# An early tile for expert 0 in a fused attention, mixture-of-experts and Fourier-mixing kernel

## What is computed

```
B, S, D, E, F = 2, 768, 512, 8, 1024         # batches, tokens, width, experts, hidden width
x = attention(q, k, v)                       # 8 heads of 64; first 8 keys and a window of 96
logits = x @ w_gate;  keep = sigmoid(x @ w_local) >= 0.5
for each batch b, for each token s in order:
    e = argmax(logits[b, s]) if s == 0 or not keep[b, s] else the expert of token s - 1
    y[b, s] = softmax(logits[b, s])[e] * (relu(x[b, s] @ w1[e]) @ w2[e])
u = y + real(fft(fft(y, over tokens), over width))
out = u + relu(normalised(u) @ w_ch1) @ w_ch2          # w_ch1: 512 x 2048
```

## Time and profile before

| what | value |
|---|---|
| median of 3 runs | 678.57 us (677.31 to 679.86) |
| the profiled execution's own time | 677.65 us |
| its span | 675.8 us |
| PE busy | 649.7 us (96%) |
| DVE, ACT, POOL busy | 317.0, 207.5, 213.7 us |
| HBM over the span | 122 GB/s |

### The profile page before, as it was taken

One profiled execution on the slowest core, in us unless ns is written; L12 is line 12 of the kernel. 1 busy time (PEld: TensorE's weight loads), 2 busy tenths in 40 slices (PEclk: granted clock), 3 DMA queues, 4 the chain that ended last, 5 costly groups with the idle time before them and its releaser, 6 DMA issues.

```text
span 675.8 us, 10507 instructions
## 1 busy us (share of the span) xinstructions
PE 649.7 (96%) x3372; PEld 530.2 (78%) x3373; DVE 317.0 (47%) x828; ACT 207.5 (31%) x410; POOL 213.7 (32%) x120
## 2 busy tenths in 40 slices
PE   8999999769999999999998989999999999999997
PEld 7777878658888888888875668888888888888886
DVE  4999787574635446345347845441221111311112
ACT  3666544303332432433204752132211122111110
POOL 0000001235778777999515646270000000000000
PEclk9999999879999999999999989999999999999999
DMA  8664347226657556678255033210010000100001
GB/s 300 245 223 165 130 132 283 81 114 236 212 166 270 191 188 243 219 243 272 64 182 163 17 125 124 94 32 0 1 62 1 1 0 1 63 0 1 0 1 62
DMA packets 35409, 82.91 MB, mean 123 GB/s; under 512 B 3362, under 2 KB 7714, under 8 KB 35364
## 3 DMA queue, kind: packets, MB, share of 16 engines
q1 hardware_dynamic: 17952, 40.46, 16.8%
q10 hardware_dynamic: 15492, 35.56, 15.9%
q0 software_dynamic: 1920, 6.29, 2.8%
HBM read 67.35 MB, written 14.94 MB: 122 GB/s over the span
## 4 chain that ended last, share of the span: by engine, by line
PE 85%; DVE 9%; issue 2%; DMA 2%; ACT 1%; POOL 0%; DVEq 0%; ACTq 0%; POOLq 0%; SPq 0%
PE psum L597 22%; PE psum L599 22%; PE psum L598 22%; PE psum L1888 5%; PE psum L1860 3%; PE psum L1871 2%; PE psum L2036 2%; PE psum L1798 2%; PE psum L1996 1%; DVE prob L1407 1%; DMA bounds_i<-in_n_local 1%; PE psum L1792 1%; DVE prob_t L1421 1%; PE psum L2117 1%; DMA u<-y_sorted,result_rows 1%
## 5 line engine op out<-in xcount | busy, mean ns | idle before, releaser
L722 POOL TENSOR_TENSOR w<-raw,w 128x1024 fp32r<-128x1024 f32 x56 | 132.5, 2398 | 40.0 <-ACT w L820 39.8
L1752 DVE SCALAR_TENSOR_TENSOR act_t<-psum,act_t 128x512 fp32r<-128x512 f32 x48 | 33.2, 691 | 191.6 <-ACT act_t L1102 191.6
L820 ACT ACTIVATE w<-raw 128x1024 fp32r<-128x1024 f32 x64 | 67.3, 1058 | 123.9 <-PE psum L599 55.7
L1102 ACT ACTIVATE act_t<-psum 128x512 fp32r<-128x512 f32 x48 | 28.7, 598 | 217.8 <-PE psum L599 217.8
L597 PE MATMUL psum<-un_t,wc 128*128 128x512 f32 x192 | 75.5, 393 | 1.4 <-DVE un_t L1676 1.4
L597 PE MATMUL psum<-wc,act_t 128*128 128x512 f32 x192 | 75.6, 394 | 0.0
L599 PE MATMUL psum<-un_t,wc 128*128 128x512 f32 x192 | 75.4, 393 | 0.0
L598 PE MATMUL psum<-un_t,wc 128*128 128x512 f32 x192 | 75.2, 392 | 0.0
L599 PE MATMUL psum<-wc,act_t 128*128 128x512 f32 x192 | 74.8, 390 | 0.0
L598 PE MATMUL psum<-wc,act_t 128*128 128x512 f32 x192 | 74.8, 389 | 0.0
L874 ACT ACTIVATE prob<-prob,top 128x256 f32<-128x256 f32 (+1 forms) x96 | 46.2, 482 | 48.1 <-DVE top L1407 47.7
(11 more groups left out here) (273 smaller groups left out, 1109.9 us busy)
## 6 DMA issues: line engine op xcount, KB each, us to landing
raw<-in_moe_w ACTq DMA_DIRECT2D x60, 512.0 KB, 4.3
k_win<-in_k SPq DMA_DIRECT2D x8, 768.0 KB, 5.6
raw<-in_moe_w_ch SPq DMA_DIRECT2D x12, 512.0 KB, 3.3
v_win<-in_v SPq DMA_DIRECT2D x8, 704.0 KB, 4.2
xs<-x_sorted SPq DMA_DIRECT2D x17, 256.0 KB, 4.6
y_sorted<-ys SPq DMA_DIRECT2D x16, 256.0 KB, 3.4
q_t<-in_q SPq DMA_DIRECT2D x8, 384.0 KB, 3.5
out<-u SPq DMA_DIRECT2D x12, 256.0 KB, 2.0
```

The source lines that it names most:

```text
L722: nc.gpsimd.tensor_tensor(w[:, slot, 1, m, at_:at_ + PIECE], raw[:, n % RING, :], w[:, slot, 0, m, at_:at_ + PIECE].bitcast(f32), ALU.subt ...
L820: nc.scalar.activation(w[:, slot, 0, m, at_:at_ + PIECE], raw[:, n % RING, :], ACT.Copy).then_inc(high_done, 1)
L1102: nc.scalar.activation(act_t[n % 2][:, 0, :], bank(act_bank(n)), ACT.Relu).then_inc(act_high, 1)
L1752: nc.vector.scalar_tensor_tensor(act_t[n % 2][:, 1, :], bank(act_bank(n)), 0.0, act_t[n % 2][:, 0, :].bitcast(f32), ALU.max, ALU.subtract) ...
```

## The change

The first 128 tokens of batch 0 for expert 0 (or all of them, if there are fewer) become tile 0. They have 128 rows of their own at the head of x_sorted, cleared at the program's start. The areas of the experts begin 128 rows later, and expert 0's area holds only what is beyond the first 128 of batch 0, and batch 1's tokens. There may be two more tiles than before (SLOTS). SP loads tile 0 as soon as batch 0's six scatters have landed (first_scattered), without the row numbers of control.

PE turns tile 0 ahead of the last two gate sums of batch 1. Its up products are put between the five routing steps of batch 1: 9 before turn_flags, 3 before ends_to_row, 3 before carry_to_column, 9 behind rank_tokens. Then come its 8 transposes and 18 of the 24 down products, 6 filler calls, the wait for the control words and 6 more. The other 6 down products stand behind the turning of tile 1. The fillers and waits that stood there before are gone, and the two register loads are behind first_up(1, 1). ACT writes the high parts and rectifies the hidden tile (first_tile_high, first_tile_hidden). DVE writes the low parts: first_tile_low ahead of the logits of batch 1, first_tile_rest inside control behind base_row, and first_tile_result copies the result after x_tile(1, 1). DVE has four more small operations in place(0), of which two are before the slots, and one in place_results. The three last gate sums have another bank, and the buffers xs, xs_t and hid0 have other places. The diff, cut to its core (the helpers turn_tile, up, first_up and tile_step of PE are moved up unchanged, but for second_product, which is taken out of tile_step):

```diff
-SLOTS = NT + E
+SLOTS = NT + E + 2
...
+    first_row = AREA * np.arange(E) + 2 * P
     row = np.concatenate([
         np.tile(slope, B),
         E - np.arange(E),
-        AREA * np.arange(E) + P,
+        np.where(np.arange(E) > 0, first_row, P),
+        first_row,
...
+    hid = [None, rc("hid1", [P, F])]
+
+    assert route_start <= rc.next and rc.next + 12288 <= rg.next
+    x2_at = rc.next
     xs = [rc(f"xs{n}", [P, DM]) for n in range(2)]
     xs_t = [rc(f"xs_t{n}", [P, 2, NC, P], f32r) for n in range(2)]
-    hid = [rc(f"hid{n}", [P, F]) for n in range(2)]
+    hid[0] = rc("hid0", [P, F])
...
-        BANK_LAST = bank(0)[:, 0:ST * (E + 1)]
+        BANK_LAST = bank(7)[:, 2 * P:2 * P + ST * (E + 1)]
...
+
+            sp.wait_ge(zeros_ready, 1)
+            sp.dma_start(x_sorted[0:P, :], zeros[:, :]).then_inc(first_tile_cleared, 16)
...
-            sp.wait_ge(zeros_ready, 1)
...
-            sp.wait_ge(rows_ready, 1)
...
-            first_rows = [row_of(j) for j in range(2)]
...
-            sp.wait_ge(scattered, 16 * NT)
-            for par in range(2):
-                load_tile(first_rows[par], par)
+            sp.wait_ge(first_scattered, 16 * ST)
+            sp.dma_start(xs[0][:, :], x_sorted[0:P, :]).then_inc(xs_loaded[0], 16)
+            sp.wait_ge(rows_ready, 1)
+            first_rows = [row_of(j) for j in range(1, 3)]
+            sp.wait_ge(scattered, 16 * ST)
+            load_tile(first_rows[0], 1)
             sp.wait_ge(xs_turned, 1)
-            load_tile(row_of(2), 0)
+            load_tile(first_rows[1], 0)
...
+            pool.wait_ge(first_tile_cleared, 16)
...
-                                        x_att[:, t, :], None).then_inc(scattered, 16)
+                                        x_att[:, t, :], None).then_inc(first_scattered if t < ST else scattered, 16)
...
+            def first_tile_high():
+                act.wait_ge(xs_turned, 1)
+                nc.scalar.activation(xs_t[0][:, 0, :, :].rearrange("p c n -> p (c n)"), bank(4), ACT.Copy
+                                     ).then_inc(xs_t_high, 1)
+
+            def first_tile_hidden():
+                for part in range(2):
+                    act.wait_ge(hid_sum, part + 3)
+                    nc.scalar.activation(hid[0][:, part * 512:(part + 1) * 512], bank(part), ACT.Relu
+                                         ).then_inc(hid_ready, 1)
+                act.wait_ge(hid_turned, 1)
+                for z in range(2):
+                    nc.scalar.activation(hid_t[:, 0, 4 * z:4 * z + 4, :].rearrange("p c n -> p (c n)"), bank(2 + z),
+                                         ACT.Copy).then_inc(hid_t_high, 1)
...
+                first_tile_high()
...
             gate_exponentials(1)
+            first_tile_hidden()
...
-            for n in range(2):
-                act.wait_ge(xs_loaded[n], 16)
+            act.wait_ge(xs_loaded[1], 16)
+            act.wait_ge(xs_loaded[0], 32)
...
+                if b == 0:
+                    link(nc.vector.tensor_scalar(in_first_tile[:, :], slot_f[:, these], 2.0 * P, float(P), ALU.is_lt,
+                                                 ALU.mult))
+                    link(nc.vector.tensor_tensor(slot_f[:, these], slot_f[:, these], in_first_tile[:, :],
+                                                 ALU.subtract))
                 nc.vector.tensor_copy(slots[:, these], slot_f[:, these]).then_inc(slots_ready, 1)
                 if b == 0:
                     link(nc.vector.tensor_tensor(area[:, :], row["area"], upto[0][:, :, ST - 1], ALU.add))
+                    link(nc.vector.tensor_tensor(area[:, :], area[:, :], row["first_row"], ALU.max))
+                    link(nc.vector.tensor_tensor(sorted_first[:, :], area[:, :], row["first_row"], ALU.subtract))
                 else:
-                    link(nc.vector.tensor_tensor(count[:, :], upto[0][:, :, ST - 1], upto[1][:, :, ST - 1], ALU.add))
+                    link(nc.vector.tensor_tensor(count[:, :], sorted_first[:, :], upto[1][:, :, ST - 1], ALU.add))
...
+                    rows = by_token[:, 0, b * ST:(b + 1) * ST]
+                    link(nc.vector.tensor_reduce(rows, cand[:, :, :], AX.X, ALU.add))
+                    if b == 0:
+                        link(nc.vector.scalar_tensor_tensor(rows, in_first_tile[:, :], 0.0, rows, ALU.is_equal,
+                                                            ALU.mult))
...
+            def first_tile_low():
+                dve.wait_ge(xs_t_high, 1)
+                flat_ = [xs_t[0][:, x, :, :].rearrange("p c n -> p (c n)") for x in (0, 1)]
+                nc.vector.tensor_tensor(flat_[1], bank(4), flat_[0].bitcast(f32), ALU.subtract
+                                        ).then_inc(xs_t_ready, 1)
+
+            def first_tile_rest():
+                for z in range(2):
+                    hi, lo = (hid_t[:, x, 4 * z:4 * z + 4, :].rearrange("p c n -> p (c n)") for x in (0, 1))
+                    dve.wait_ge(hid_t_high, z + 1)
+                    nc.vector.tensor_tensor(lo, bank(2 + z), hi.bitcast(f32), ALU.subtract).then_inc(hid_t_ready, 1)
+
+            def first_tile_result():
+                dve.wait_ge(mm2_parts, 2 * PARTS)
+                nc.vector.tensor_copy(ys[0][:, :], bank(5)).then_inc(ys_ready, 1)
...
-                link(v.scalar_tensor_tensor(base_row[:, :], last_tile[:, :], float(-P), row["area"], ALU.mult, ALU.add))
+                link(v.tensor_tensor_scan(last_tile[:, :], ones[:, 0:E], tiles[:, :], 1.0, ALU.mult, ALU.add))
+                link(v.scalar_tensor_tensor(base_row[:, :], last_tile[:, :], float(-P), row["first_row"], ALU.mult,
+                                            ALU.add))
                 link(v.tensor_tensor(base_row[:, :], base_row[:, :], count[:, :], ALU.add))
+                first_tile_rest()
...
-            x_tile(0, 0)
+            x_tile(1, 1)
+            first_tile_result()
             share(1)
             first_results()
-            x_tile(1, 1)
-            rectify(0, 0, 0)
-            rectify(0, 0, 1)
-            tile_step(0, 0, 2)
+            x_tile(2, 0)
+            rectify(1, 1, 0)
+            rectify(1, 1, 1)
+            tile_step(0, 1, 2)
             mirrored_rows()
-            tile_step(0, 1, 2)
             with dve.Fori(1, HALVES_LEAST - 1) as p:
...
+            pe.sem_inc(hid_sum, 2)
+            pe.sem_inc(mm2_parts, PARTS)
...
+            def second_product(par, slot, c):
+
+                ins = three_passes(bank(5 + par), hid_t[:, 0, c, :], hid_t[:, 1, c, :],
+                                   weights(slot, 0, 1, c * DM), weights(slot, 1, 1, c * DM), c == 0, c == NF - 1)
+                if c % 2 == 1:
+                    ins.then_inc(mm2_parts, 1)
...
-                for t in range(4):
+                for t in (2, 3, 0, 1):
                     sum_last(t)
                 values(UNITS - 1)
                 pe.wait_ge(x_unit_done, UNITS)
                 turn_x(len(X_FILLS) - 1)
+                turn_tile(0, 0, 16)
...
-            for stage in (turn_flags, ends_to_row, carry_to_column, codes_to_columns, rank_tokens):
-                stage(1)
...
-            pe.wait_ge(slots_ready, 2)
-            keep_busy(7)
-            pe.wait_ge(rows_ready, 1)
-            keep_busy(8)
...
+            pe.wait_ge(rest_done, WPIECES // 2)
+            pe.wait_ge(xs_t_ready, 1)
+            up(0, 0, 0, 0, range(NC - 1))
+            turn_flags(1)
+            up(0, 0, 0, 0, range(NC - 1, NC))
+            ends_to_row(1)
+            up(0, 0, 1, 0, range(1))
+            carry_to_column(1)
+            codes_to_columns(1)
+            rank_tokens(1)
+
+
+            pe.wait_ge(rest_done, WPIECES)
+            up(0, 0, 1, 0, range(1, NC))
+            for z in range(2):
+                pe.wait_ge(hid_ready, z + 1)
+                for c in range(4):
+                    ins = nc.tensor.transpose(bank(2 + z)[:, c * P:(c + 1) * P],
+                                              hid[0][:, (4 * z + c) * P:(4 * z + c + 1) * P], ident)
+            ins.then_inc(hid_turned, 1)
+            for c in range(NF - 2):
+                if c % 4 == 0:
+                    pe.wait_ge(hid_t_ready, c // 4 + 1)
+                second_product(0, 0, c)
+            keep_busy(6)
             pe.wait_ge(ctl_ready, 1)
+            keep_busy(6)
...
-            keep_busy(7)
-            turn_tile(0, 0, 16)
-            keep_busy(3)
-            first_up(0, 0)
             turn_tile(1, 1, 16)
-            up(0, 0, 1, slot_of(0))
+            for c in range(NF - 2, NF):
+                second_product(0, 0, c)
+            first_up(1, 1)
+            half = HALVES_LEAST + nc.tensor.value_load(ctl[0:1, CTL_MORE], min_val=0, max_val=SLOTS // 2 - HALVES_LEAST)
+            odd = nc.tensor.value_load(ctl[0:1, CTL_ODD], min_val=0, max_val=1)
+            turn_tile(2, 0, 32)
+            up(1, 1, 1, slot_of(1))
             mirror_rows()
-            first_up(1, 1)
-            tile_step(0, 0, 2)
+            first_up(2, 0)
```

(1 more changed line is left out.)

161 lines of the change are left out of this document (80 added, 81 removed).

## The result

Over 19 runs each on one chip the kernel before took 677.51 us (676.12 to 679.86) and the kernel after 683.04 us (677.07 to 685.99). The ratio is 1.0062, with a 95% interval of 1.0045 to 1.0079. The change costs about half a per cent where a gain of 8.9 us was forecast. No set of runs shows a gain.

The account below looks back on a forecast made before the run. PE was taken to bound the kernel (85% of 675.8 us). 12.3 us leaving the packed stretch, less 1.2, 2.0, 0.1 and 0.1, gave 8.9 us gained: 669.7 us, range 665.5 to 673.5.

Parts of the forecast that it names:

- rival (2): Clock stays down through the whole routing hole of batch 1: d = 2.6, gain 6.5 us, 672.1 us; chance 0.17.
- The wait inside control: VectorE waits behind base_row for both halves of the early hidden tile, making the control words 2.2 us later.
- rival (3): Batch 0's tile or expert 1's weights land late; 2 us late gives 671.7 us; chance 0.07.
- the cover of 0.7 us: Batch 0's tile is in SBUF at 128.5 and PE turns it at 129.2; lateness beyond that counts fully.
- Rival (4): Slower: expert 0's split costs a 17th tile, 12.3 us on PE, giving 682.0 us; chance 0.03.
- rival (5): The early tile's work waits until routing is over and all is only reordered: about 678.6 us; chance 0.04.
- cases 1 to 3 and the forecast: The first three rivals plus the forecast with d = 2.0, together the chance of faster, given as 0.92.
- d: Delay of batch 1's five routing steps by the up products put between them; taken as 2.0 us.
- rival (1): Clock stays up or returns at once in the routing hole: d = -0.2, gain 11.1 us, 667.5 us; chance 0.28.
- VectorE subtracts (0.69) to 131.0, before the logits are there: End of attention: the low part of tile 0 on VectorE was to delay batch 1's chain by nothing.
- the cover of 1.8: Tile loop's start: tile 2 is split 4.9 us after tile 1's first product, PE needs it at 6.65 us.
- The four small operations in place(0): VectorE's extra operations around batch 0's slots, 0.24 us each: 0.1 us taken, bounded by 0 and 0.9.

Follow-up runs that it names:

- before_share_late: The kernel before, with share(1) and first_results moved behind x_tile(1, 1), among POOL's subtractions; ratio to the kernel before 1.0173 (1.0069 to 1.0276).
- ports_clear: The kernel after, with share(1) moved into control and first_results ahead of x_tile(1, 1), before POOL's first subtraction; 675.41 us, ratio to the kernel before 0.9923.
- low_outside: The kernel after, with first_tile_low moved behind attention's If/Else instead of at the branch's end, PE untouched; ratio to the kernel before 1.002 (0.9977 to 1.0063).
- second_version: The kernel after, reordered: first_tile_low behind choose_fresh(1), three up products between flags and ends, hidden split after control words, share(1) and first_results earlier; 671.1 us, 0.9847 of before.
- before_late_branch: The kernel before, with a VectorE wait for the last gate sums added at the end of attention's branch; ratio to the kernel before 1.005 (1.0008 to 1.0092).
- products_behind: The kernel after, with all up products of the early tile moved behind the routing steps (behind rank_tokens); ratio to the kernel before 1.0107 (1.0087 to 1.0127).
- share_early: The kernel after, with share(1) moved from behind x_tile(1, 1) into control, ahead of first_tile_rest; 675.61 us, ratio to the kernel before 0.9927 (0.9894 to 0.996).
- after_again: The kernel after, unchanged, run once more for a second profile; 681.58 us, one run.

## Why the prediction was wrong, step by step

**Right.** The tile left: 16 stores, and turnings 12.3 us apart. The granted clock is back by 143 to 144 us, so rival (2) is out. The wait inside control: 2.2 was worked out, 2.11 came. From the control words to the first product 5.8 us were worked out (151.8 to 157.6), and 5.80 came (156.18 to 161.98). The loads of rival (3) held: PE waits neither for xs nor for expert 1's weights, and the cover of 0.7 us was enough. Rival (4), a 17th tile, didn't come. Nor did rival (5): the early tile's work stands in the hole, where it was to stand. One slip of arithmetic has no weight: the chances of cases 1 to 3 and the forecast add up to 0.93, not 0.92.

**Right by luck.** For d, the price of the nine products, 2.0 was taken. The copy of the flags grew by 2.26, and with the -0.19 of the shorter small steps after it that is 2.07 in all; the spacing in the rows is the 0.43 foreseen. But two premises failed, and the errors cancelled. The clock was to fall behind the attention tail, as before. It stayed up over that tail, as rival (1) had it, and fell only in PE's gap of 3.18 us, which the sum didn't have. And the products started 2.76 us later than assumed (134.06 against 131.3), which would have cost that much more, had not the logits, and with them the flags' readiness, been 2.56 us late as well. Whether the clock would have stayed up without the gap, no run shows.

**The step that failed.** "Tile 1's VectorE work now has first_tile_result (0.69), share(1) and first_results (11 small operations, 2.2 us) between the splits of tiles 1 and 2 ... hidden by 1.8." The count was right and the durations were those of the kernel before, where POOL was idle at that time. Moved behind x_tile(1, 1), they begin 6.2 us later (162.29 against 156.11), while POOL's first subtraction moved by 4.4 (163.04 against 158.60), and they meet. The four operations took 8.84 us instead of 0.71. The 8.1 us more, less the cover of 1.8, give about 6.3. The ledger has 7.42. By PE's rows 5.5 of it is the wait for the hidden tile (5.42 us in the row), 1.4 the half clock of the six products behind it, and 0.5 a later start behind the turning of tile 2 (165.72), which is not assigned. before_share_late shows the mechanism in a kernel without the change, and ports_clear shows its removal in the one with it. The prediction asked of the moved operations how long they are and whom they delay. It didn't ask which engine is at work at their new place, and it listed no such rival.

**The second step.** "VectorE subtracts (0.69) to 131.0, before the logits are there": priced at nothing, cost 1.97 us. The logits were not late because their sums were late, but because the branch had just been left. first_tile_low moved the end of the branch's last instruction from 0.29 to 2.57 us behind the start of the last write of x_att, and the gap of 2.27 came after. (The subtraction itself, forecast to end at 131.0, ended at 131.59.) PE's gap before its first product (3.18 us) has no price in the sum either: the products were taken to start at 131.3 and started at 134.06. For the flags this second gap counts, not the first (low_outside); both are repaired only if the flags' turning goes first and VectorE's branch ends early (second_version: flags at 5.87 against 5.46). Why leaving the branch takes so long is not proven, but the traces point to the loading of instructions. In the kernel after, the two instruction queues of the DMA carry 47 packets in the whole span, and two of them just here:

```profile
q8 instruction: 1, 0.02, 7.6%
q14 instruction: 1, 0.01, 3.3%
```

This is the window 131 to 132 us. In half-microsecond windows the first of the two falls in 131.0 to 131.5, behind PE's last gate sum (ends at 130.88), and the second in 131.5 to 132.0, where first_tile_low ends (131.59). In the kernel before, q14 has its packet at 129.0 to 129.5, behind the last write of x_att; in before_late_branch at 134.5 to 135.0, behind the added wait. That q8 loads for PE and q14 for VectorE is inferred from this order. The Trainium skill (Runtime: NRT & Kernel Launch, Instruction fetch mechanics) says that a taken branch whose target is outside the fetched part of the program has to fetch it first. It gives no price, and the runs show 2.2 to 2.9 us on VectorE. PE's gap ahead of the up products was 2.8 to 3.2 us, but in the kernel before PE left its branch and stood ready for the flags within 2.55 us (130.71 to 133.26), so PE's gap is not all a fixed price of the branch; the rest of it is open.

**A term that was too small.** The four small operations in place(0) were taken at 0.1 with 0.9 as the bound. The write of x_att that follows them (the 43rd) stands at 117.23 us in the kernel before and at 118.09 in the kernel after, 0.86 late: the upper bound. 0.59 of it is left at the end. No run isolates it, though PE has a gap of 0.41 us ahead of the gate products at 118.49 there which the kernel before doesn't have.

**The sum again.** The packed stretch starts 5.53 us later: 0.59 at the end of attention, 1.97 behind the branch, and 2.97 for d and what follows it (2.26 - 0.19 + 2.11 - 1.21), where 3.2 was predicted. With 7.42 for the small operations that is 12.3 - 5.53 - 7.42 = -0.65, a loss by 179 us where 8.9 us of gain were forecast. The profiled executions differ by 678.61 - 677.65 = 0.96 at the end. In between, PE waited 1.57 us for a weight piece of POOL:

```profile
313.30 0.49 PE L608 MATMUL psum<-w,xs_t 128*128 x1 [1.57 <-POOL w L736]
```

Such a wait of PE for POOL's piece stands in each profile of the kernel after (1.57, 1.27 and 1.3 us), in products_behind (0.6) and in low_outside (0.8), and in none of share_early, ports_clear, second_version and the kernel before. So it goes with the late start of the packed stretch's second tile in the kernels with the change; by what path wasn't isolated. Against that, the kernel before has seven products at half clock at 396 to 399 us, worth 7 x 0.2 = 1.4 us, and the kernel after has none: 0.65 + 1.57 - 1.4 = 0.8 of the 0.96. POOL had a gap of 2.1 us between expert 1's and expert 2's pieces where none was forecast; PE waited for neither.

**The median, and what stays open.** The median of the kernel after is 4.4 us above its profiled execution. Its three profiles differ in the end of attention: the last write of x_att is at 129.02, 132.36 and 131.05. From there to the end they take 549.6, 549.2 and 551.5 us, and the kernel before takes 549.2. So what lies behind attention costs the change 0 to 2.3 us, and as far as single profiles tell, the rest of the 5.5 us between the medians lies in attention. The rows of PE show where. In after_again:

```profile
125.71 0.36 PE L1864 MATMUL psum<-gate_w,x_t 128*128 128x9 f32 x2 [1.96 <-issue]
```

PE stands still for 1.96 us ahead of two gate products in the last units of attention, waiting for nothing that the profile shows. In that profile 1.3 us more follow at half clock (0.63 granted from 126 to 128 us and 0.52 from 128 to 130), which makes the 3.3 us. The same gap, ahead of the same two products, stands in seven of the eight profiles of kernels with the early tile (1.94 to 2.18 us; not in the first one), and in both variants of the kernel before (1.40 and 1.41 us), but not in the one profile of the kernel before itself. It isn't the loading of instructions of the kind seen behind the branch: in after_again no packet of the instruction queues falls between 118 and 132 us. So the gap belongs to both kernels. Whether the change makes it more frequent, which would carry the loss in the median, or only longer, and what causes it, is open. The 0.86 us at the 43rd write is there in each profile of the kernel after (118.09, 118.11 and 118.12, against 117.23 and 117.21 in the kernel before and in before_share_late).

## What to carry to other kernels

When a step of VectorE with operands in SBUF is moved in time, look at what POOL does at the new time, and not only at the operations around it: where POOL works over whole tensors, each small operation with two inputs in SBUF, and each small tensor_scalar, cast or copy there, can cost up to one of POOL's instructions. Order them ahead of POOL's stretch. (Letting them read PSUM instead is a way that no run here tried.) In the trace of the kernel at hand, look for a small operation of ten times its usual length that ends with one of POOL's. And a branch's last instruction is not a free slot: what stands behind the branch starts 2.2 to 2.9 us later than it.
